# MLP weights in order of use, the second expert block's tokens turned inside the first up projection, and the last product in a bank of its own

## The reference

```python
# 1: windowed attention with a distance bias, 4 x 8 heads, head size 64
scores = np.where((rel >= 0) & (rel < 128), scale * q @ k.T + bias, -1e9)
x = softmax(scores) @ v                       # heads joined: (4, 576, 512)
# 2: Fourier mixing and an MLP of width 2048
u = x + np.real(fft(fft(x, axis=1), axis=2))
un = (u - mean(u)) / sqrt(var(u) + 1e-6)
x = u + maximum(un @ w_ch1, 0) @ w_ch2        # (512, 2048), (2048, 512)
# 3: 8 experts of width 1024, one for each token
fresh = argmax(x @ w_gate); e = fresh where sigmoid(x @ w_local) < 0.5, else the one before
out = p[e] * (maximum(x @ w1[e], 0) @ w2[e])
```

## Time and profile before

| | before |
|---|---|
| median of 3 runs | 969.17 us (968.7 to 970.1) |
| the profiled execution | 969.82 us, its span 968.0 us |
| mean granted clock of TensorE | 0.974 |
| TensorE matmuls busy | 906.0 us |
| VectorE busy | 458.8 us |

### The profile page before, as it was taken

One profiled execution on the slowest core, in us unless ns is written; L12 is line 12 of the kernel. 1 busy time (PEld: TensorE's weight loads), 2 busy tenths in 40 slices (PEclk: granted clock), 3 DMA queues, 4 the chain that ended last, 5 costly groups with the idle time before them and its releaser, 6 DMA issues.

```text
span 968.0 us, 22638 instructions
## 1 busy us (share of the span) xinstructions
PE 906.0 (94%) x9128; PEld 639.6 (66%) x9129; DVE 458.8 (47%) x843; ACT 308.8 (32%) x425; POOL 282.9 (29%) x298
## 2 busy tenths in 40 slices
PE   5899998899999999999999999974899999999995
PEld 2566666556767677676767676743777777777772
DVE  4788887564624242424233333656975777000000
ACT  3677767343321111111112121220223332233331
POOL 2466776310101010101111010001344544334431
PEclk9899999899999999999999999986999999999998
DMA  8255542524311010101010100521765665111110
GB/s 289 63 160 171 144 156 73 161 77 136 97 37 41 27 43 22 43 22 43 22 43 22 43 22 22 174 66 42 224 225 189 202 218 160 53 40 43 43 32 0
DMA packets 55342, 89.24 MB, mean 92 GB/s; under 512 B 7140, under 2 KB 26035, under 8 KB 55165
## 3 DMA queue, kind: packets, MB, share of 16 engines
q1 hardware_dynamic: 49853, 72.56, 24.1%
q0 software_dynamic: 5440, 16.00, 5.3%
HBM read 71.19 MB, written 16.55 MB: 91 GB/s over the span
## 4 chain that ended last, share of the span: by engine, by line
PE 83%; DVE 8%; DMA 3%; issue 3%; SPq 1%; ACT 1%; POOL 0%; DVEq 0%; POOLq 0%; ACTq 0%
PE psum L804 20%; PE psum L821 19%; PE psum L989 13%; PE psum L974 13%; PE psum L599 4%; PE psum L743 3%; PE psum L755 2%; DVE m_mem L1254 2%; DVE arena L1282 2%; PE psum L944 1%; DMA m_mem<-in_qk 1%; DMA m_mem<-x_rows,m_mem 1%; PE psum L654 1%; PE psum L673 1%; PE psum L765 1%
## 5 line engine op out<-in xcount | busy, mean ns | idle before, releaser
L804 PE MATMUL psum<-m_mem,arena 128*128 (+1 forms) x1728 | 198.8, 273 | 0.3 <-DVE arena L1514 0.3
L821 PE MATMUL psum<-arena,m_mem 128*128 128x512 f16 x864 | 195.3, 379 | 0.0
L804 PEld LDWEIGHTS psum<-m_mem,arena 128*128 128x128 f16 x1728 | 168.3, 98 | 26.1 <-DVE arena L1514 0.6
L974 PEld LDWEIGHTS psum<-m_mem,arena 128*128 x2400 | 138.9, 98 | 9.3 <-issue 3.8
L974 PE MATMUL psum<-m_mem,arena 128*128 128x128 f16 x2400 | 141.0, 220 | 3.6 <-ACT m_mem L1192 3.6
L821 PEld LDWEIGHTS psum<-arena,m_mem 128*128 128x128 f16 x864 | 84.5, 98 | 90.5
L989 PE MATMUL psum<-arena,m_mem 128*128 x600 | 133.6, 379 | 1.2 <-ACT m_mem L1214 1.2
L1127 ACT ACTIVATE m_mem<-psum 128x512 f16<-128x512 f32 x72 | 43.0, 597 | 251.3 <-PE psum L804 250.3
L989 PEld LDWEIGHTS psum<-arena,m_mem 128*128 128x128 f16 x600 | 57.6, 98 | 66.6 <-issue 1.7
L1422 DVE SCALAR_TENSOR_TENSOR m_mem<-psum,m_mem 128x512 f16<-128x512 f32 x72 | 49.8, 691 | 103.0 <-ACT m_mem L1127 103.0
L1759 POOL TENSOR_TENSOR arena<-m_mem,arena 128x1024 f16<-128x1024 f32 x9 | 18.0, 1995 | 272.2 <-ACT arena L1142 227.2
(11 more groups left out here) (217 smaller groups left out, 1064.5 us busy)
## 6 DMA issues: line engine op xcount, KB each, us to landing
dimdft_sb<-in_exp_w SPq DMA_DIRECT2D x74, 256.0 KB
wstage<-in_exp_w SPq DMA_DIRECT2D x54, 256.0 KB, 2.9
m_mem<-in_qk SPq DMA_DIRECT2D x16, 576.0 KB, 4.6
arena<-in_v SPq DMA_DIRECT2D x32, 160.0 KB, 4.4
x_rows<-m_mem SPq DMA_DIRECT2D x16, 320.0 KB, 3.3
x_rows<-arena SPq DMA_DIRECT2D x9, 512.0 KB, 2.8
wstage<-in_mlp_w SPq DMA_DIRECT2D x16, 256.0 KB, 3.2
arena<-in_mlp_w SPq DMA_DIRECT2D x16, 256.0 KB, 2.9
```

The costliest lines, as they stand in the source:

```text
L804: last = nc.tensor.matmul(psum[:, 2 + k % 4, (f % 2) * 2 * P:(f % 2 + 1) * 2 * P], w1_sb[:, sp_, c, f * P:(f + 1) * P], unT[:, bass.ds(t % ...
L821: last = nc.tensor.matmul(psum[:, 6 + q, :], hT[:, k % 4, sp_, at:at + P], w2_sb[:, mp, f, :], start=f == 0 and sp_ == 0 and mp == 0, stop ...
L974: last = nc.tensor.matmul(psum[:, 2 + f // 4, f % 4 * P:(f % 4 + 1) * P], pointed(regs[wp * EW + c * FE + f * P], P), xeT[:, mp, c, :], st ...
```

## The change

Three things change at once.

The MLP's chunks are loaded and converted in the order `W_ORDER`, in which the MLP's steps use them: w_ch1's columns for steps 0 and 1, those for 2 and 3, four chunks of w_ch2, and so on. Only 8 chunks, in place of 16, are converted inside the spectrum stage, each one place later than before: none stands after the very first spectrum chunk. The other 20 go to tile 0 (3, 3, 3, 3, 4, 4 in steps 0 to 5). The waits of `hidden` and `project` in tile 0 name the count that each needs.

Block 1's tokens are turned in the middle of `up(0)`, ahead of its seventh of eight groups; their copy goes to a buffer of its own (the memory of `ye`, not in use yet) and stands on ScalarE ahead of `relu(0)`; `up(1)` writes banks 4 and 5, and `relu(1)` reads them. `gather_block(2)` moves on GpSimd ahead of `he_lo_of(0)`.

`down(24)` writes bank 7, does not wait for `weigh(23)`, and `weigh(24)` reads bank 7.

```diff
+PER_F = FF // CH
+W_UP = [[c * PER_F + g for c in range(DC)] for g in range(PER_F)]
+W_DOWN = [DC * PER_F + f for f in range(FF // P)]
+W_ORDER = W_UP[0] + W_UP[1] + W_DOWN[0:4] + W_UP[2] + W_DOWN[4:8] + W_UP[3] + W_DOWN[8:]
+W_SPEC = 4
+W_DFT = 8
+W_TILE0 = [3, 3, 3, 3, 4, 4, 0, 0]
+def w_count(chunks):
+    return max(W_ORDER.index(n) for n in chunks) + 1
+def w_tile0(k):
+    at = W_SPEC + W_DFT + sum(W_TILE0[0:k])
+    return range(at, at + W_TILE0[k])
...
-                sp.dma_start(w_staging[n % WRING], mlp_w[n]).then_inc(w_loaded[n % WRING], 16)
+                sp.dma_start(w_staging[n % WRING], mlp_w[W_ORDER[n]]).then_inc(w_loaded[n % WRING], 16)
...
-            W_TOP = W_SPEC + DC * B
+            W_TOP = W_SPEC + W_DFT
...
-                if first and k == 0:
-                    pe.wait_ge(w_split, DC * FF // CH)
+                if first and k % 2 == 0:
+                    pe.wait_ge(w_split, w_count(W_UP[k // 2]))
...
-                    pe.wait_ge(w_split, DC * FF // CH + 2 * k + 2)
+                    pe.wait_ge(w_split, w_count(W_DOWN[2 * k:2 * k + 2]))
...
-            def up(k, e, slot, first):
+            def up(k, e, slot, first, second):
...
-                if not first:
+                if not first and not second:
                     pe.wait_ge(hs_done, k)
+                tokens, bank = (xeT_second, 4) if second else (xeT, 2)
                 for f in range(FE // P):
+                    if first and f == 6:
+                        transpose_xe(1)
...
-                if not first:
+                if not first and not last_bank:
                     pe.wait_ge(ye_done, k)
...
-                        last = nc.tensor.matmul(psum[:, 6, :], heT[:, turn, sp_, f, :],
+                        last = nc.tensor.matmul(psum[:, 7 if last_bank else 6, :], heT[:, turn, sp_, f, :],
...
-                if not last:
+                if not first and not last:
                     transpose_xe(k + 1)
...
-                    w_hi_of(W_SPEC + DC * b + c)
+                    if 0 < DC * b + c <= W_DFT:
+                        w_hi_of(W_SPEC + DC * b + c - 1)
...
-                    for n in range(W_SPEC + DC * B + 2 * k, min(WCH, W_SPEC + DC * B + 2 * k + 2)):
+                    for n in w_tile0(k):
                         w_hi_of(n)
...
             def experts(k, first=False, second=False, last=False):
-                relu(k, first, first or second)
-                if not last:
+                if first:
+                    copy_xeT(k + 1, second=True)
+                relu(k, first, first or second, bank=4 if second else 2)
+                if not first and not last:
                     copy_xeT(k + 1)
...
-            weigh(NBLK - 1, False)
+            weigh(NBLK - 1, False, bank=7)
...
-                if n == W_FREE:
+                at = W_ORDER[n]
+                if at >= W_FREE and n == min(W_ORDER.index(i) for i in range(W_FREE, WCH)):
                     dve.wait_ge(x_split, PAIRS)
                     dve.wait_ge(table_made, 2)
...
-                    w_lo_of(W_SPEC + DC * b + c)
+                    if 0 < DC * b + c <= W_DFT:
+                        w_lo_of(W_SPEC + DC * b + c - 1)
...
+                if first:
+                    gather_block(k + 2)
                 he_lo_of(k)
-                if ahead > 1:
+                if not first and ahead > 1:
                     gather_block(k + 2)
```

More of the change, by code:

```diff
@@ L65 @@
 ECH = EW // CH
-assert WCH == 2 * DC * B and ECH == 2 * (MT - 1)
+assert ECH == 2 * (MT - 1)
+PER_F = FF // CH
+W_UP = [[c * PER_F + g for c in range(DC)] for g in range(PER_F)]
+W_DOWN = [DC * PER_F + f for f in range(FF // P)]
+W_ORDER = W_UP[0] + W_UP[1] + W_DOWN[0:4] + W_UP[2] + W_DOWN[4:8] + W_UP[3] + W_DOWN[8:]
+assert sorted(W_ORDER) == list(range(WCH))
+W_SPEC = 4
+W_DFT = 8
+W_TILE0 = [3, 3, 3, 3, 4, 4, 0, 0]
+assert W_SPEC + W_DFT + sum(W_TILE0) == WCH
+def w_count(chunks):
[3 more added lines that the diff above has]
+    return range(at, at + W_TILE0[k])
 NSLOT = 4
@@ L205, in fused_kernel @@
         W_FREE = (xsh_at - w_at - W_WORDS // 2) // CH
-        W_SPEC = 4
         rows_at = w_at + W_WORDS
@@ L973, in up @@
                         for wp, mp in THREE:
-                            last = nc.tensor.matmul(psum[:, 2 + f // 4, f % 4 * P:(f % 4 + 1) * P],
-                                                    pointed(regs[wp * EW + c * FE + f * P], P), xeT[:, mp, c, :],
+                            last = nc.tensor.matmul(psum[:, bank + f // 4, f % 4 * P:(f % 4 + 1) * P],
+                                                    pointed(regs[wp * EW + c * FE + f * P], P),
+                                                    tokens[:, mp, c, :],
                                                     start=c == 0 and wp == 0 and mp == 0,
@@ L978, in up, with down @@
                 last.then_inc(eh_ready, 1)
-            def down(k, turn, slot, first=False):
+            def down(k, turn, slot, first=False, last_bank=False):
                 pe.wait_ge(he_lo, k + 1)
-                if not first:
+                if not first and not last_bank:
                     pe.wait_ge(ye_done, k)
@@ L1002, in experts @@
                     _, last_slot = expert_of(k - 1)
-                up(k, e, slot, first)
-                if not last:
+                up(k, e, slot, first, second)
+                if not first and not last:
                     transpose_xe(k + 1)
@@ L1020, in _ @@
             _, slot = expert_of(NBLK - 1)
-            down(NBLK - 1, 0, slot)
+            down(NBLK - 1, 0, slot, last_bank=True)
         @block.scalar
@@ L1187, in _, with copy_xeT, relu @@
             nc.scalar.activation(pex, dl, ACT.Exp).then_inc(exp_ready, 1)
-            def copy_xeT(k):
+            def copy_xeT(k, second=False):
                 act.wait_ge(xeT_ready, k + 1)
-                nc.scalar.activation(xeT.rearrange("p i c s -> p (i c s)"), psum[:, 0, :].bitcast(F16), ACT.Copy)\
+                nc.scalar.activation((xeT_second if second else xeT).rearrange("p i c s -> p (i c s)"), psum[:, 0, :].bitcast(F16), ACT.Copy)\
                     .then_inc(xeT_copied, 1)
-            def relu(k, first, early):
+            def relu(k, first, early, bank=2):
                 act.wait_ge(eh_ready, k + 1)
@@ L1807, in scatter_block, with experts @@
                                              bounds_check=TOK - 1, oob_is_err=False).then_inc(out_stored, 16)
-            def experts(k, ahead=2, scatter=True):
+            def experts(k, ahead=2, scatter=True, first=False):
                 if scatter:
@@ L1823, in _ @@
             for k in range(2):
-                experts(k, scatter=False)
+                experts(k, scatter=False, first=k == 0)
             with pool.Fori(2, NBLK - 2) as k:
```

16 lines of the change are left out of this document (9 added, 7 removed).

## The result

| | after |
|---|---|
| median | 959.77 us (959.02 to 960.6, 4 runs), before 969.15 us in the same comparison |
| ratio to before | 0.9901, 95% interval 0.9884 to 0.9919 |
| the profiled execution | 960.6 us, its span 958.6 us |
| mean granted clock of TensorE | 0.981 |

The kernel became 9.4 us faster, 2.4 less than the forecast said. The spans differ by 968.0 - 958.6 = 9.4 us too, so two timelines can be set side by side and must account for that number.

The account below looks back on a forecast made before the run. TensorE, busy for 94% of the span, was taken as the bound; gains of 5.5 + 5.45 + 1.2 and 0.2 more, less 0.6 lost, made 11.8 us, taking the median from 969.17 to 957.4 us, range 955.3 to 961.0.

Parts of the forecast that it names:

- Part 1: First spectrum chunks: idle 2.49 us ahead of chunk 3 goes and the clock returns (3.03), 5.5 us gained together.
- the cover of 0.6 us: Spectrum chunk 1: VectorE's split ends at 176.3, TensorE wants chunk 3 at 176.9; enough for one conversion colliding with GpSimd.
- clock term: Spectrum stage: the 54 matmuls behind the gap take 7.97 us at full clock instead of 11.00, another 3.03 us gained.
- Part 2: MLP tile 0, now with 20 chunks in place of 12: 0.3 us lost, ends 0 and 1.5.
- The collisions that the prediction feared there: Tile 0, after `fold`: two more conversions beside GpSimd's half of the residual; if both collided, 1.1 us later.
- Part 3: Block 1's tokens: `up(0)` to `down(0)` shrinks from 17.17 us to 11.72, 5.45 gained, 0.3 lost for two gathers.
- both blocks run so: 11.72: Blocks 0 and 1: each `up` with its transposes takes the steady blocks' 5.86 us, 11.72 us for both.
- 3.0 are the wait, 1.6 the clock: Split of block 1's 5.45 us gain: 3.0 wait, 1.6 clock, the rest the wait for block 2's gather.
- the gathers of blocks 1 and 2 come late: Rival for the first blocks: 1.0 us and as much again, 1.7 more than taken, 959.1 us; chance 0.05.
- Part 4: Last block: `down(24)` no longer waits for `weigh(23)`, 1.2 us gained, bounds 0 and 1.2; block 24's record fits by 1.3.
- The clock cost moves rather than goes: Rival: the 1.78 us gap behind the spectrum stage stays and may lower the clock; 3.0 us back, 960.4; chance 0.12.

## Why the forecast was right in its kind and 2.4 us too low

The mechanisms were the forecast ones: the gaps go, the clock comes back where they go, and the three parts add up. The median, 959.77, lies inside the range and nearer its high end. By the steps of the prediction:

- **Part 1, 5.5 us and 0.2.** Mis-sized. The profiled stretch gave 4.55. The step that failed is the cover of 0.6 us, "enough for one conversion that collides": beside GpSimd the two conversions were longer than in the trace of before by 0.4 us together and the gate's operations by 0.4 and 0.8, 1.6 in all, and 1.18 us of the gap stayed. Its clock term was right for this pair of traces (7.94 us, forecast 7.97), but by luck in its size: it took one execution's 3.03 for a fixed price, and in three others it was 1.5. Against the mean of these three and of the trace of before, 17.70 us from chunk 1 to the edge product, the kernel after gains 3.3 us, and 4.5 to 4.6 where the rest of the gap is gone as well.
- **Part 2, 0.3 lost.** Mis-sized in the safe direction: no wait in tile 0; 0.16 us longer over all of the MLP and the routing. The cover shrank to 0.5 us, forecast 0.2. The collisions that the prediction feared there (1.1 us) did not come: the four conversions between `fold` and `normalise_u` took 0.64 us each.
- **Part 3, 5.45 less 0.3.** The profiled stretch gave 4.67. The gathers of blocks 1 and 2 cost nothing, so the 0.3 wasn't due. Failed is "both blocks run so: 11.72": that pace holds behind a `down`, where the reading of registers is covered; between two `up`s it took 0.8 us more, of which 0.61 is the idle stretch of the reading. Wrong in its ground, though not in the sum, was "3.0 are the wait, 1.6 the clock": the 1.6 was there in two of five traces, and where it was absent it came back as a wait for the gather.
- **What the sum did not have: 1.26 us, nearly all for block 4.** The prediction followed the gathers of blocks 1 and 2 and stopped. With block 1 done 4.7 us sooner, GpSimd's scatter, record and gather for the next blocks get no more time than before, and meet the weight loads; over the eight kernels TensorE's wait is 0.75 us on average. The rival "the gathers of blocks 1 and 2 come late" did not happen as it was put; another gather of the same kind was late, at a like price.
- **Part 4, 1.2.** Right: 1.36 in the trace, and the record of block 24 wasn't late.
- **The rivals.** "The clock cost moves rather than goes" did not happen: the slow edge product is there before and after alike, and with or without the change in other kernels. That a gap costs differently from one execution to the next was seen in all three: 3.0 us once and 1.5 in three ahead of chunk 3, 1.6 in two and 0 in three ahead of `up(1)`, 1.5 to 1.7 in seven and 0 in four ahead of the edge product. The Trainium skill, TensorE: Matmul & The Clock Gate, Part 1, says that the monitor's time doesn't restart with the kernel; these numbers are in line with that, though no run here shows that it is the reason.

From 11.75 forecast (5.7 - 0.3 + 5.15 + 1.2) to 9.38: 1.15 less in part 1, 0.14 more in part 2, 0.48 less in part 3, 1.26 less for block 4, 0.16 more in part 4 and 0.22 more from the attention, which the change doesn't touch.

## What to carry to other kernels

When a stage is pulled forward, follow what was waited for until it is steady again, not just to the next two transfers: what stood behind a stall had its slack from it. A clock loss read from one execution is one draw; take it from several executions, or fill the gap once to see whether the time depends on it at all. And a small operation is no small risk when it stands between a copy and its reader beside a busy neighbour: move it out of the way rather than count on its usual length.

## What the runs showed of the hardware

- A VectorE operation on 36 numbers a partition with two inputs in SBUF took 0.20 us with no arithmetic of GpSimd beside it, 0.52 to 0.57 beside GpSimd instructions of 0.63 to 0.69, and 1.33 beside one of 1.39, which it ended with. The Trainium skill, SBUF — State Buffer, Who interferes with whom, says that a VectorE instruction with two SBUF inputs contends with a GpSimd instruction that reads SBUF; the trace agrees. So here the price followed the neighbour's length and not its own. GpSimd paid too: the fold's half beside the conversions and the gate's first operation took 1.08 us in place of 0.63.
- An idle stretch of TensorE of 1.8 us was followed by a stretch at lower clock in seven traces and by full clock in four; with that stretch filled by matmuls without use, the clock stayed full in all three.
- Reading a second block's expert and slot into TensorE's registers ahead of `up(0)`, where nothing was queued, lengthened the idle stretch there from 0.55 to 0.59 us to 1.25. Behind a `down`, of 5.34 us, such a reading cost nothing.
- One gather of 128 rows took 3.3 to 3.4 us from issue to landing as the first of the stage, and 4.7 to 6.7 us among the weight loads where TensorE waited for it.
